# ScalarE scales six of twelve tiles, the first unit of layer one is reordered, and the first parts of head 0 are made by halves in place

## The reference

```python
def _attn_ref(q, k, v, proj):              # 2 batches, 8 heads, 768 tokens, head size 64
    q_bits = (einsum('bhsd,dk->bhsk', q, proj) > 0)      # 6 bits each, k_bits alike
    mask = q_bucket[..., :, None] == k_bucket[..., None, :]
    scores = where(mask, scale * (q @ k.T), -1e9)
    attn = softmax(scores)
    return attn @ v
x = attention output as (1536, 512)
x = ((x @ w1) * (x @ w2)) @ w3 @ w_out                          # d_ff 1024
out = (sigmoid(x @ w_gate) * (x @ w_val)) @ moe2_w_out          # d_ff 1536
```

## Time and profile before

| what | value |
|---|---|
| median of 3 runs | 775.24 us (774.24 to 775.75) |
| the profiled execution: its time | 775.34 us |
| the profiled execution: its span | 773.3 us |
| busy: TensorE matmul, weight load | 731.5 us (95%), 675.3 us (87%) |
| busy: VectorE, ScalarE, GpSimd | 480.9 (62%), 456.2 (59%), 345.2 us (45%) |
| chain that ended last, by engine | PE 74%, DVE 13%, issue 6%, ACT 4%, DMA 2% |
| mean granted TensorE clock | 0.995 of full speed |

### The profile page before, as it was taken

The page is one execution under the profiler, slowest core; times in us unless marked ns, Lnnn a source line. Parts: engine busy times, 40 slices in busy tenths (PEclk is TensorE's granted clock), DMA queues, the critical chain, the costliest instruction groups (busy, mean ns, idle before and its releaser), DMA issues.

```text
span 773.3 us, 12684 instructions
## 1 busy us (share of the span) xinstructions
PE 731.5 (95%) x4136; PEld 675.3 (87%) x4136; DVE 480.9 (62%) x1032; ACT 456.2 (59%) x842; POOL 345.2 (45%) x253
## 2 busy tenths in 40 slices
PE   6798989899898989799999999999999999999998
PEld 4687878778797878799999999999999999988886
DVE  5899999999999999832432833624324326774100
ACT  5788888897888988545446424564454454715100
POOL 3867364554628697164466600054653554140000
PEclk9999999999999999999999999999999999999999
DMA  5774443436273500001001000010010010401001
GB/s 154 219 175 105 116 124 94 129 89 165 71 175 91 115 12 18 28 28 56 28 27 54 1 0 1 1 55 28 28 54 28 27 55 0 163 1 68 28 28 41
DMA packets 26609, 51.79 MB, mean 67 GB/s; under 512 B 4161, under 2 KB 12689, under 8 KB 26577
## 3 DMA queue, kind: packets, MB, share of 16 engines
q1 hardware_dynamic: 26272, 51.32, 24.4%
q10 hardware_dynamic: 304, 0.07, 0.0%
HBM read 29.43 MB, written 3.15 MB: 42 GB/s over the span
## 4 chain that ended last, share of the span: by engine, by line
PE 74%; DVE 13%; issue 6%; ACT 4%; DMA 2%; SPq 1%; DVEq 0%; ACTq 0%
PE pair_bank L1296 14%; PE pair_bank L1298 14%; PE pair_bank L1297 13%; PE bank L1296 5%; PE bank L1298 5%; PE bank L1297 5%; PE bank L1224 5%; PE bank L1209 5%; PE pair_bank L1197 4%; DVE pt_lo L957 4%; DVE rowmax L924 4%; ACT pt_hi L617 2%; DMA qk_raw<-in_qk 2%; DVE prob L949 1%; PE bank L1258 1%
## 5 line engine op out<-in xcount | busy, mean ns | idle before, releaser
L1062 DVE TENSOR_TENSOR u<-bank,u 128x384 f32<-128x384 f32 x80 | 44.3, 555 | 135.5 <-ACT u L617 126.6
L617 ACT ACTIVATE u<-pair_bank 128x384 f32<-128x384 f32 x120 | 58.7, 491 | 109.3 <-PE pair_bank L1298 109.1
L1209 PEld LDWEIGHTS bank<-ident,prob 128*128 128x128 f32 x576 | 65.8, 141 | 49.7 <-DVE pt_lo L957 29.7
L1209 PE MATMUL bank<-ident,prob 128*128 128x128 f32 x576 | 85.3, 281 | 24.9 <-DVE pt_lo L957 24.3
L617 ACT ACTIVATE pt_hi<-bank 128x384 fp32r<-128x384 f32 x192 | 85.8, 489 | 32.2 <-PE bank L1209 31.7
L957 DVE TENSOR_TENSOR pt_lo<-bank,pt_hi 128x384 fp32r<-128x384 f32 x192 | 97.4, 548 | 7.8 <-ACT pt_hi L617 7.5
L650 ACT ACTIVATE prob<-pair_bank,ebias,escale 128x768 f32<-128x768 f32 x96 | 95.1, 991 | 7.2 <-DVE ebias L935 7.0
L924 DVE TENSOR_REDUCE rowmax<-pair_bank 128x1 f32<-128x768 f32 x96 | 90.9, 947 | 4.2 <-PE pair_bank L1197 4.0
L1197 PE MATMUL pair_bank<-mk,sq 128*128 128x384 f32 x384 | 89.7, 356 | 3.6 <-ACT prob L650 1.9
L1296 PE MATMUL pair_bank<-y_hi,g_hi 128*128 128x384 f32 x240 | 80.3, 335 | 0.0
L1197 PEld LDWEIGHTS pair_bank<-mk,sq 128*128 128x128 f32 x384 | 65.2, 191 | 8.8 <-issue 6.2
(11 more groups left out here) (162 smaller groups left out, 1953.6 us busy)
## 6 DMA issues: line engine op xcount, KB each, us to landing
sq<-hl SPq DMA_DIRECT2D x45, 192.0 KB
mk<-hl SPq DMA_DIRECT2D x15, 384.0 KB
qk_raw<-in_qk SPq DMA_DIRECT2D x7, 768.0 KB, 5.6
w_raw<-in_w SPq DMA_DIRECT2D x16, 256.0 KB, 2.7
v_raw<-in_v SPq DMA_DIRECT2D x16, 192.0 KB, 2.7
wo_raw<-in_wo SPq DMA_DIRECT2D x12, 256.0 KB, 3.6
out<-out_sb SPq DMA_DIRECT2D x12, 256.0 KB, 2.0
mk<-hl SPq DMA_DIRECT2D x15, 192.0 KB
```

The costliest lines, as they stand in the source:

```text
L617: return act.activation(dst, src, ACT.Copy)
L1209: mm = pe.transpose(t_bank[j][:, 128 * t:128 * t + 128], prob[k % 3][:, 128 * (3 * j + t):128 * (3 * j + t) + 128], ident[:, :])
```

## The change

Five edits.

1. **Scaling.** `NORM_ON_ACT` is now a list of steps: 2, 3, 5, 8, 9, 11. Steps 3 and 9 move from VectorE to ScalarE.
2. **Program start.** ScalarE and GpSimd write the high parts of head 0 by halves straight into `sq[0]` and `mk[0]`, VectorE subtracts straight into them, and `first_parts` counts to 12. `hl`, from now on only needed for head 1, is made later, by halves; its last half stands behind the first row maximum. `WARM` is 10 and 14. SyncE waits for `first_parts` and issues the load of pair 1 ahead of the five copies. GpSimd's `v_split(0, 0)` waits for `first_parts` too.
3. **Pair 0.** `bits(1)` stands at step 3 and `code(1)` at step 4.
4. **B22 and the first unit.** GpSimd makes both parts of B22 in the last pair, behind T3's high part. ScalarE no longer has B22.
5. **T4 in two steps.** Its early half is subtracted on VectorE as soon as attention ends (`x_sum4_begin`); T2's other half is copied by ScalarE (`x_take_t2`), so that T2's low part need not wait for the last output. The orders of both engines in the first unit change accordingly.

The diff, without the declarations of new semaphores and the places where only a count of ten becomes twelve:

```diff
-WARM = (10, 30)
-NORM_ON_ACT = (2,)
+WARM = (10, 14)
+NORM_ON_ACT = (2, 3, 5, 8, 9, 11)
...
-X_HI_ORDER = ((T2, 0), (T2, 1), (T1, 0), (T1, 1), (B22, 0), (B21, 0), (B22, 1), (T4, 0), (B21, 1), (T4, 1))
-X_LOW_ORDER = ((T3, 0), (T3, 1), (T2, 0), (T1, 0), (T2, 1), (T1, 1), (B22, 0), (B22, 1), (B21, 0), (B21, 1),
-               (T4, 0), (T4, 1))
+X_HI_ORDER = ((T2, 0), (T2, 1), (T1, 0), (T1, 1), (B21, 0), (B21, 1), (T4, 0), (T4, 1))
+X_LOW_ORDER = ((T3, 0), (T3, 1), (T2, 0), (T2, 1), (T1, 0), (T1, 1), (B21, 0), (B21, 1), (T4, 0), (T4, 1))
...
-            sp.wait_ge(hl_ready, 1)
+            sp.wait_ge(first_parts, 12)
+            load_qk(1, 1, 1)
             assemble_parts(1)
-            sp.wait_ge(first_parts, 10)
-            load_qk(1, 1, 1)
...
+                    pool.wait_ge(s_done, STEPS * PAIRS)
+                    for side in range(2):
+                        rounded(x_high(B22, side), x_raw(B22, side)).then_inc(x_hi_early, 1)
+                    for side in range(2):
+                        pool.wait_ge(x_hi_early, side + 5)
+                        pool.wait_ge(x_sums_done, side + 5)
+                        pool.tensor_tensor(x_low(B22, side), x_raw(B22, side), x_high(B22, side).bitcast(F32),
+                                           ALU.subtract).then_inc(x_low_early, 1)
...
-            pool.wait_ge(qk_first, 16)
-            pool.wait_ge(qk_loaded, 16)
-            rounded(mk[0][0:D, 0:1, :], qk_raw[0:D, 1:2, :], zeros[0:D]).then_inc(first_parts, 1)
+            for hf, loaded in enumerate((qk_first, qk_loaded)):
+                cols = slice(HALF * hf, HALF * hf + HALF)
+                pool.wait_ge(loaded, 16)
+                rounded(mk[0][0:D, 0:1, cols], qk_raw[0:D, 1:2, cols], zeros[0:D]).then_inc(first_k, 1)
+            pool.wait_ge(first_parts, 12)
             v_split(0, 0)
...
-                if q in (T1, B22):
+                if q == T1:
...
+                    act.wait_ge(x_sum4_begun, 1)
...
+            def x_take_t2():
+                act.wait_ge(x_sums_done, 4)
+                act.wait_ge(wp_done, PAIRS)
+                copy(x_sums[T4][0][:, :, 1, :], x_sums[T2][0][:, :, 1, :]).then_inc(x_t2_taken, 1)
...
-                    if k % UQ in NORM_ON_ACT:
+                    if k in NORM_ON_ACT:
...
-            act.wait_ge(qk_first, 16)
-            copy(hl[:, 0::2, 0:HALF], qk_raw[:, :, 0:HALF])
-            act.wait_ge(qk_loaded, 16)
-            copy(hl[:, 0::2, HALF:SEQ], qk_raw[:, :, HALF:SEQ]).then_inc(qk_hi_done, 1)
-            copy(mk[0][D:2 * D, 0, :], qk_raw[0:D, 1, :]).then_inc(first_parts, 1)
-            copy(sq[0][0:D, 0, :], qk_raw[0:D, 0, :]).then_inc(first_parts, 1)
-            copy(sq[0][0:D, 1, :], qk_raw[0:D, 0, :]).then_inc(first_parts, 1)
+            def first_high(hf):
+                cols = slice(HALF * hf, HALF * hf + HALF)
+                return copy(hl[:, 0::2, cols], qk_raw[:, :, cols])
+            for hf, loaded in enumerate((qk_first, qk_loaded)):
+                cols = slice(HALF * hf, HALF * hf + HALF)
+                act.wait_ge(loaded, 16)
+                copy(sq[0][0:D, 0, cols], qk_raw[0:D, 0, cols]).then_inc(first_q, 1)
+                copy(sq[0][0:D, 1, cols], qk_raw[0:D, 0, cols]).then_inc(first_parts, 1)
+                copy(mk[0][D:2 * D, 0, cols], qk_raw[0:D, 1, cols]).then_inc(first_parts, 1)
+            first_high(0).then_inc(first_hi, 1)
...
             act.wait_ge(codes_done, 1)
...
+            first_high(1).then_inc(qk_hi_done, 1)
...
+            x_take_t2()
...
             kept1(0, 0, 1, u_x)
+            x_operand_high(T1, 1)
             attention_halves(3, PAIRS - 1, keep=False)
-            x_operand_high(T1, 1)
-            x_operand_high(B22, 0)
+            kept2(0, 0, 0, u_x)
             x_operand_high(B21, 0)
-            kept2(0, 0, 0, u_x)
-            x_operand_high(B22, 1)
             kept2(0, 0, 1, u_x)
+            x_operand_high(B21, 1)
             kept4(0, 0, 0, u_x)
+            kept4(0, 0, 1, u_x)
             x_operand_high(T4, 0)
-            kept4(0, 0, 1, u_x)
-            x_operand_high(B21, 1)
-            gate(ACT.Copy, 0, 0, y4_mm, 0, 0, y_bank[0], g12_done)
             x_operand_high(T4, 1)
-            gate(ACT.Copy, 0, 1, y4_mm, 0, 0, y_bank[1], g12_done)
+            for side in range(2):
+                gate(ACT.Copy, 0, side, y4_mm, 0, 0, y_bank[side], g12_done)
             pair_sums_high(1, 1)
...
-                if q in (T2, B21):
+                if q == T2:
+                    dve.wait_ge(x_sums_done, 5 + side)
+                    dve.wait_ge(x_sum4_begun, 1)
+                    dve.wait_ge(x_t2_taken, 1)
+                if q == B21:
+                    dve.wait_ge(x_sum4_begun, 1)
...
-                if q in (T2, B22):
-                    dve.wait_ge(x_sums_done, 5 + side)
...
+            def x_sum4_begin():
+                dve.wait_ge(x_done, 2 * (PAIRS - 1))
+                dve.wait_ge(x_sums_done, 4)
+                dve.wait_ge(wp_done, PAIRS)
+                dve.tensor_tensor(x_sums[T4][0][:, :, 0, :], x_f[:, PAIRS - 2, :].rearrange("p (s n) -> p s n", s=2),
+                                  x_sums[T2][0][:, :, 0, :], ALU.subtract).then_inc(x_sum4_begun, 1)
...
+                late = x_sums[T4][0][:, side, 1, :]
...
-                dve.wait_ge(x_sums_done, 3 + side)
-                dve.wait_ge(wp_done, PAIRS)
-                dve.tensor_tensor(x_raw(T4, side), x_raw(B21, side), x_raw(T2, side),
+                dve.wait_ge(x_t2_taken, 1)
+                dve.tensor_tensor(late, x_f[:, PAIRS - 1, HALF * side:HALF * side + HALF], late,
...
-                    if k % UQ not in NORM_ON_ACT:
+                    if k not in NORM_ON_ACT:
...
-                    if k == 2 and not last:
+                    if k == (4 if first else 2) and not last:
...
+            for hf in range(2):
+                cols = slice(HALF * hf, HALF * hf + HALF)
+                dve.wait_ge(first_q, hf + 1)
+                dve.tensor_tensor(sq[0][D:2 * D, 0, cols], qk_raw[0:D, 0, cols], sq[0][0:D, 0, cols].bitcast(F32),
+                                  ALU.subtract).then_inc(first_parts, 1)
+                dve.wait_ge(first_k, hf + 1)
+                dve.tensor_tensor(mk[0][0:D, 1, cols], qk_raw[0:D, 1, cols], mk[0][0:D, 0, cols].bitcast(F32),
+                                  ALU.subtract).then_inc(first_parts, 1)
             code(0)
-            dve.wait_ge(qk_hi_done, 1)
-            dve.tensor_tensor(hl[:, 1::2, :], qk_raw[:, :, :], hl[:, 0::2, :].bitcast(F32),
-                              ALU.subtract).then_inc(hl_ready, 1)
...
-            dve.wait_ge(hl_ready, 1)
-            dve.tensor_copy(sq[0][D:2 * D, 0, :], hl[0:D, 1, :].bitcast(F32)).then_inc(first_parts, 1)
-            dve.tensor_copy(mk[0][0:D, 1, :], hl[0:D, 3, :].bitcast(F32)).then_inc(first_parts, 1)
+            def first_low(hf):
+                cols = slice(HALF * hf, HALF * hf + HALF)
+                return dve.tensor_tensor(hl[:, 1::2, cols], qk_raw[:, :, cols], hl[:, 0::2, cols].bitcast(F32),
+                                         ALU.subtract)
+            dve.wait_ge(first_hi, 1)
+            first_low(0)
             row_max(0, 0)
...
             exp_bias(0, 0)
+            dve.wait_ge(qk_hi_done, 1)
+            first_low(1).then_inc(hl_ready, 1)
...
-            dve.wait_ge(x_done, 2 * (PAIRS - 1))
+            x_sum4_begin()
+            x_operand_low(T2, 0)
+            x_operand_low(T2, 1)
...
             attention_out(slice(0, 2 * D), 0, x_f[:, PAIRS - 1, 0:HALF])
             x_sum4(0)
-            x_operand_low(T2, 0)
             x_operand_low(T1, 0)
+            x_operand_low(T1, 1)
             attention_out(slice(0, D), 1, x_f[0:D, PAIRS - 1, HALF:SEQ])
...
             x_sum4(1)
-            for q, side in X_LOW_ORDER[4:10]:
-                x_operand_low(q, side)
+            x_operand_low(B21, 0)
+            x_operand_low(B21, 1)
...
-                    if k == 1 and not last:
+                    if k == (3 if first else 1) and not last:
...
+                elif q == B22:
+                    pe.wait_ge(x_low_early, side + 3)
```

8 lines of the change are left out of this document (5 added, 3 removed).

## The result

The changed kernel is slower: 782.39 us (median of 19 runs, 777.37 to 786.25) against 775.99 us (19 runs, 773.76 to 781.70), a ratio of **1.0077, 95% interval 1.0061 to 1.0093**. The forecast was 773.9, in a range from 768.0 to 778.9, so it was wrong in sign and the measured time is outside the range. The profiled execution took 782.39 us (span 780.6, mean granted clock 0.985, where before had 0.995).

The account below looks back on a forecast made before the run. TensorE's waits at the program start with pair 0, in the pairs and in the first unit were taken as the bound. +0.9 - 0.5 - 1.8 = -1.4 from 775.34 gave 773.9 us, range 768.0 to 778.9.

Parts of the forecast that it names:

- The queue of the two engines: Everywhere: a VectorE instruction reading SBUF twice, or scaling prob, waits while GpSimd runs one, ending some 0.35 behind it.
- The pairs: Six loop pairs: moving two scalings to ScalarE gains 0.1 us each, -0.5 in all; bounds -1.8 and +0.65 a pair.
- the loss of 0.1 at step 10: Loop pairs, step 10: ScalarE's high parts start later, mostly covered by GpSimd's v_st; 0.1 of step 4's 0.2 gain remains.
- The rule on the highest occupancy: Pairs: VectorE, 97% busy, is the bound, so 1.24 to 1.76 a pair returns: 763 to 766 us; rival, chance 0.10.
- The slower rival: Pairs, step 10: ScalarE becomes the bound, each of seven pairs pays 0.65 and more, 4.6: 778.7 us; chance 0.17.
- Pair 0: Program start and pair 0: first scores 2.6 us earlier, but GpSimd's late qk_split(1) leaves only 0.3 at the first fill.
- The term of +0.9: Program start and pair 0: 0.3 gained, 1.2 lost to lower clock behind a new 3 us wait; bounds -4 and +2.5.
- The warm-up: Program start: the shorter warm-up ends 1 us before the scores; costed at nothing, a clock drop if that cover is gone.
- The first unit: First unit of layer one: 7.1 us of losses replaced by 5.3, a gain of 1.8; bounds -6.1 and +0.5.
- the late start: Start of the first unit: step 9's scaling, uncovered in the last pair, makes the unit start at 304.5, 0.85 later.
- T1: First unit: VectorE's instructions queue behind GpSimd's sums, so T1 is ready at 316.1, due at 314.2: 1.95.
- The rivals together: Chances: no first-unit queue 0.15, VectorE bound 0.10, pair 0 keeps gain 0.08, ScalarE bound 0.17, loads and copies slower 0.08.

Follow-up runs that it names:

- e1: The changed kernel with the scaling of steps 3 and 9 back on VectorE: 779.09 us, 1.0022 of the kernel before.
- e5: e4 with step 3's scaling alone also moved to ScalarE: 777.37 us, 1.0030 of the kernel before.
- e4: The kernel before with only the B22, T4 and first-unit order edits: 773.64 us, 0.9965 of the kernel before.
- e3: The changed kernel with five more matmuls put into step 4's wait in pairs 1 to 7: 777.49 us, 1.0007 of the kernel before.
- e15: e5 with the five added matmuls of e3 in front of step 4's wait: 772.27 us, 0.9951 of the kernel before.
- e6: e4 with step 9's scaling alone also moved to ScalarE: 775.41 us, 1.0000 of the kernel before.
- e7: e1 with the warm-up back to 30 transposes instead of 14: 780.71 us, 1.0062 of the kernel before.
- e9: e4, old program start, with weights loaded and split ahead of qk_split(1), bits(1) at step 3, code(1) at step 4: 776.95 us, 1.0006 of the kernel before.
- e2: The changed kernel with the old program start, warm-up and pair 0's bits and codes: 778.27 us, 1.0019 of the kernel before.
- e11: e1 with weights loaded and split first, and hl's second half made ahead of the first row maximum: 772.72 us, 0.9958 of the kernel before.
- e12: e1 with weights loaded and split first, step 3's scaling on ScalarE and e3's five matmuls: 771.55 us, 0.9935 of the kernel before.
- e13: e12 with hl's second half also made ahead of the first row maximum: 770.49 us, 0.9934 of the kernel before.

## Why the prediction was wrong, point by point

- **What bounds the kernel** was read rightly: TensorE's waits in three places decide, and all three moved. The queue of the two engines was read rightly too: the scaling at 178.61 took 2.60 for the reason given there.
- **The pairs: the length was right, the clock was left out.** The forecast had pairs of 35.4; in the changed kernel the wait at step 4 stands at 109.36 in pair 2 and 144.76 in pair 3, 35.40 apart, with no drop in between. The 0.2 at step 4 and the loss of 0.1 at step 10 are there as well (0.22 and 0.09 in the row maxima), but for pair 6, where step 10 loses 0.8 (below). The step that failed is "the transposes of step 4 go at 175.45 instead of 175.65: 0.2 gained". It looked at when the wait ends, not at how long TensorE then stands idle in one piece: the 1.04 of step 3 did not vanish, it moved behind step 4's. I priced a drop of the clock in pair 0 and in the first unit, and not in the one place that comes six times. In its place the runs showed 4.3 us lost by the whole scaling edit (after against e1), 5.1 by step 3 alone (e5 against e4), and none once the wait is filled (e3, e15). (The Trainium skill, TensorE: Matmul & The Clock Gate, HAM oscillation — how this bites in real kernels, describes this: a wait repeated in a loop puts the engine back to the lower clock each time round. Here it was so in four of six pairs in two executions and in one of six in a third, so less often than each time round.)
- **The rule on the highest occupancy** (the Trainium skill, Perfetto Trace Analysis, Identifying the Most-Contended Engine) did not hold here: shortening VectorE's work at step 3 by 1.24 gave 0.2 a pair where the wait was filled (e15), and a loss where it was not (e5). The rows' reading was right against it.
- **The slower rival** had 0.17 and 778.7 (773.9 + 4.6 is 778.5). Its size for the scaling, 4.6, was near the 4.3 measured. Its mechanism, ScalarE late at step 10, is seen in one pair of the seven, pair 6, for 0.8 us (e6); the other pairs of the loop are 0.1 longer. Right size for a mostly wrong reason, which is luck.
- **Pair 0.** First scores at 11.20 for 10.4 (VectorE stood in front of `shift`, its wait ends at 6.52, and the subtractions queue behind it), `qk_split(1)` at 26.60 for 25.4, the first fill at 38.83 for 37.4: the chain was right and 1.2 to 1.4 short. The step that failed is the count of the waits behind it. "The same list holds up the load of wo1 ... that costs no more than it already loses" was wrong: before, ScalarE did not wait for it; now it waits 3.01, which became the 2.56 at step 4. Head 1's own first scores, which also stand behind the copies that start later, were left out: 1.72. And the list of the next pair was not followed: SyncE's copies of pair 1 stand behind GpSimd's split of the w3 tile, which ended at 36.05, and pair 1's first scores waited for them. Four waits where one was priced, and two drops at them where one was priced; a third drop stands at 14 to 20, behind a wait of 1.90 for the first exponential that before has too (1.91, no drop). The term of +0.9, with bounds of -4 and +2.5, measured +4.4 (+6.2 by itself).
- **The warm-up** was costed at nothing, and a shorter one was not the loss: e7 is 3 us worse with the long one, which ended behind the first operands. A length between 14 and 30 was not tried.
- **The first unit: right in sign, too small.** Forecast -1.8 with the late start in it; measured -2.7 for the edits alone (e4, which has no late start), and 3.85 - 0.86 = 3.0 gained in the trace of the changed kernel. The late start is 0.86 for 0.85, the values 0.91 for 1.35, B22 0.95 for 1.15. T1 was mis-sized: 0.50 for 1.95 (1.05 in e4). Of the four instructions that I took for queued, costing 3.6 more than free ones, only T2's two were much so, 3.73 for 1.82; T1's own two took 1.82, since GpSimd stood idle from 322 on. The forecast also had the step 9 scaling cost 0.85 behind the loop; with pair 6's step 10 it is 1.6 (e6).
- **The rivals together**: each looked for one place where the change goes wrong. It went wrong in two at once, and each alone would have eaten the first unit's gain.

## What to carry to other kernels

When work is moved off an engine in front of a wait, ask whether two short waits of TensorE become one long one: here the sum of its waits fell from 2.74 to 2.42 a pair while the time rose. Where such a wait can't be removed, try redundant matmuls in it that end before it does. They cost nothing here (e3, e15), and show at once whether the clock is the cause. An earlier start is worth only what passes the last door of that stage: list all waits behind it, on into the next iteration's transfers, and move the idle engine's work into its idle time, unless another engine's instructions would stand behind it there, as VectorE's did behind GpSimd's in e9.

## What the runs showed of the hardware

- Whether the clock drops behind a given wait differs between executions of one kernel: a joined wait of 1.75 was followed by a drop in four of six pairs in two profiled executions and in one of six in a third; waits of 1.04 and 1.33 with work between them by none in any profile. One drop costs 1.56 us.
- The length of the wait alone does not decide it. Step 4 of the last pair has one wait of 1.68 to 1.70 in eleven profiles, before among them, and the end of attention one of 1.79 to 1.82 in four (after, e2, e3, e6); none of these fifteen was followed by a drop. What sets them apart from the joined wait in the loop stays open. The one in before:

```profile
281.88 0.92 PE L1209 MATMUL bank<-ident,prob 128*128 128x128 f32 x6 [1.68 <-DVE pt_lo L957]
```

- Four kernels without the joined wait (e11) or with it filled (e12, e13, e15) have all their runs within 1.3 us, 6 to 10 runs each. Others without it (e1, e4, before) scatter by 3 to 8 in 12 to 19 runs. Their profiles are at full clock between 60 and 310 us, so pair 0 is the likely place; that is argued, not shown, and what makes the difference there was not told apart.
- In the program start the lower clock lasted up to 17 us in one piece (e9, from 16 to 33), far longer than behind a wait in the loop.
- Five added matmuls of 128 x 512 took 0.23 each in the wait (1.16 from the first of them to the next instruction), and moved nothing.
- VectorE's plain copies stand behind GpSimd too: a copy of 64 x 768 took 1.51 and 2.58 beside its work (e9), and 0.55 in before.
